# Fused delta-rule attention and two expert layers on one core: the Gram products moved ahead of the state's products in each group

## What is computed

```python
k_n = k / (norm(k) + 1e-6)
state = zeros((B, H, D, D))
for t in range(S):
    kt, vt, bt = k_n[:, :, t], v[:, :, t], beta[:, :, t, None]
    y[:, :, t] = einsum('bhd,bhde->bhe', q[:, :, t], state)
    v_old = einsum('bhde,bhd->bhe', state, kt)
    state = state + bt[..., None] * einsum('bhd,bhe->bhde', kt, vt - v_old)
```

## Time and profile before

| what | value |
|---|---|
| median of three runs | 1571.28 us |
| the profiled execution, its time | 1558.92 us |
| its span, from first to last instruction | 1557.2 us |
| mean granted TensorE clock, share of 2.4 GHz | 0.943 |
| TensorE busy | 1369.3 us, 88% |
| VectorE, ScalarE, GpSimd busy | 504.3, 479.6, 380.8 us |
| keep-busy products (line 960) | 192, 326 ns each (median) |
| starts of the transposes (line 993) in two neighbouring groups at full clock | 334.38 and 357.98 us |
| attention stage | 38 to 662 us |
| gated layer | 687 to 1134 us |
| routing, then the experts | 1134 to 1189, then to 1557 us |

### The profile page before, as it was taken

The page is one execution under the profiler, slowest core; times in us unless marked ns, Lnnn a source line. Parts: engine busy times, 40 slices in busy tenths (PEclk is TensorE's granted clock), DMA queues, the critical chain, the costliest instruction groups (busy, mean ns, idle before and its releaser), DMA issues.

```text
span 1557.2 us, 27716 instructions
## 1 busy us (share of the span) xinstructions
PE 1369.3 (88%) x10241; PEld 1096.6 (70%) x10242; DVE 504.3 (32%) x1030; ACT 479.6 (31%) x1159; POOL 380.8 (24%) x360
## 2 busy tenths in 40 slices
PE   4788888888888898869999999999915999999997
PEld 4677877777777787758888888888802555555554
DVE  1666555555565556421111111111130111111111
ACT  1454546354445454432222222212110111111110
POOL 4323222233232323112231223221242111111111
PEclk9789899899998989989999999999957999999999
DMA  3221000000000000060000000000092223331110
GB/s 120 67 67 32 22 27 22 27 22 27 23 27 22 27 22 27 7 221 1 1 1 1 1 0 0 0 0 1 0 352 111 73 77 107 119 110 37 32 30 6
DMA packets 39475, 72.75 MB, mean 47 GB/s; under 512 B 3946, under 2 KB 27538, under 8 KB 39377
## 3 DMA queue, kind: packets, MB, share of 16 engines
q1 hardware_dynamic: 33872, 55.50, 10.7%
q0 software_dynamic: 5504, 15.77, 3.0%
HBM read 55.50 MB, written 17.13 MB: 47 GB/s over the span
## 4 chain that ended last, share of the span: by engine, by line
PE 76%; DVE 9%; issue 6%; ACT 3%; POOL 2%; DMA 2%; DVEq 0%; SPq 0%; ACTq 0%; POOLq 0%
PE ps L1067 19%; PE ps L1131 11%; PE ps L1142 10%; PE ps L1078 10%; DVE BA L526 3%; PE ps L980 3%; PE ps L1010 3%; PE ps L1002 2%; PE ps L936 2%; DVE MP L545 2%; PE ps L935 2%; PE ps L1151 2%; PE ps L916 2%; DVE CT L536 1%; POOL xs_dram L469 1%
## 5 line engine op out<-in xcount | busy, mean ns | idle before, releaser
L1067 PE MATMUL ps<-xh,wgh 128*128 128x512 f32 x432 | 170.7, 395 | 12.7 <-DVE wol L624 7.0
L449 POOL TENSOR_TENSOR gl<-gp,gh 128x512 fp32r<-128x512 f32 x72 | 93.0, 1291 | 349.6 <-ACT gh L833 349.6
L636 DVE TENSOR_TENSOR gp<-sg,ps 128x512 f32<-128x512 f32 x72 | 49.5, 688 | 385.0 <-PE ps L1067 384.1
L1067 PE MATMUL ps<-xl,wgh 128*128 128x512 f32 x432 | 170.3, 394 | 0.0
L1131 PE MATMUL ps<-W,xsT 128*128 x372 | 168.6, 603 | 1.9 <-ACT xsT L884 1.0
L1067 PE MATMUL ps<-xh,wgl 128*128 128x512 f32 x432 | 169.8, 393 | 0.0
L1142 PE MATMUL ps<-W,hT 128*128 x496 | 165.1, 486 | 0.9 <-ACT hT L880 0.9
L545 DVE TENSOR_TENSOR MP<-ps,mE 128x256 f16<-128x256 f32 x288 | 115.5, 421 | 136.9 <-PE ps L1002 133.4
L1142 PEld LDWEIGHTS ps<-W,hT 128*128 128x128 f32 x496 | 94.2, 190 | 73.0 <-issue 15.5
L762 ACT CAST Xs<-ps 128x256 f16<-128x256 f32 x288 | 109.6, 381 | 98.4 <-PE ps L1010 92.8
L428 POOL TENSOR_TENSOR lof<-CT,BA 128x512 f32<-128x512 f16 x48 | 62.5, 1301 | 264.0 <-DVE CT L536 264.0
(11 more groups left out here) (177 smaller groups left out, 2446.2 us busy)
## 6 DMA issues: line engine op xcount, KB each, us to landing
W<-w_dram SPq DMA_DIRECT2D x16, 1536.0 KB, 11.0
kv<-kv_dram SPq DMA_DIRECT2D x24, 384.0 KB, 3.1
xs_dram<-zrow SPq DMA_DIRECT2D x1, 6076.0 KB, 22.0
xs<-xs_dram POOLq DMA_DIRECT2D x31, 196.0 KB, 2.7
kqT<-qT_dram SPq DMA_DIRECT2D x48, 96.0 KB, 2.5
XX<-woT_dram SPq DMA_DIRECT2D x1, 2304.0 KB, 9.9
stage<-w_gate_dram SPq DMA_DIRECT2D x6, 384.0 KB, 3.7
stage<-w_val_dram SPq DMA_DIRECT2D x6, 384.0 KB, 3.2
```

The source lines that it names most:

```text
L449: pool.tensor_tensor(gl[f % 2][:, :], gp[f % 2][:, :], gh[f % 2][:, :].bitcast(F32), ALU.subtract).then_inc(gl_ok, 1)
L636: nc.vector.tensor_tensor(gp[f % 2][:, :], sg[f % 2][:, :], ps[2 + f % 2][:, :], ALU.mult).then_inc(gp_ok, 1)
L1067: mm = pe.matmul(s[:, :], w[:, m, a, cols], v[par][:, a, :], start=(a == 0 and x == 0), stop=(a == KT - 1 and x == 2))
```

## The change

In every body that has a front and a rear, TensorE issues the Gram products first, and `keys_state(0)` and `keys_state(1)` behind them. `weights_w(0)` moves behind the transposes of the first half, `weights_w(1)` behind those of the second half. On VectorE, Rp moves from ahead of the maskings to behind the first half's XTs. All eight keep-busy products of a body are gone from there; `keep_warm` is called nowhere else. The closing body keeps its order, without keep-busy products.

```diff
--- before.py
+++ after.py
@@ -518,7 +518,7 @@
                     ins = nc.vector.tensor_tensor(sv, sv, ps[7][rows, 0:NPAIR * D].rearrange("p (h d) -> p h d", d=D), ALU.add)
                 ins.then_inc(st_ok, 1)
 
-            if cg is not None:
+            if cg is not None and g is None:
                 keys_state()
             if g is not None:
                 for j in range(4):
@@ -537,6 +537,8 @@
                         wait(dve, ct_ok, 2 * g + hf + 1)
                         wait(dve, xx_ps, 16 * g)
                         nc.vector.tensor_tensor(XTs[:, hs, :], CT[:, hs, :], mL[:, :].unsqueeze(1).to_broadcast([P, 4, P]), ALU.mult).then_inc(xt1_ok, 1)
+                        if hf == 0 and cg is not None:
+                            keys_state()
             if g is not None:
                 for l in range(1, LEVELS):
                     for hf in range(2):
@@ -965,11 +967,9 @@
                     for f, *a in chain.get((l, x), ()):
                         f(*a)
 
-            if cg is not None:
+            if cg is not None and g is None:
                 keys_state(0)
-                keep_warm(2, 0)
                 keys_state(1)
-                keep_warm(2, 0)
             if g is not None:
                 wait(pe, kT_ok, 2 * g + 2)
                 wait(pe, q_in[par], 32 * (base // 2) + 32 * (k // 2 + 1))
@@ -980,11 +980,12 @@
                         mm = pe.matmul(ps[j][:, 256 * s:256 * s + 256], kbT[:, p, r, :],
                                        kqT[par][:, p, :, :].rearrange("p a t -> p (a t)"), start=True, stop=True)
                     mm.then_inc(gram_ps, 1)
-            if cg is not None:
+            if cg is not None and g is not None:
+                keys_state(0)
+                keys_state(1)
+            if g is None:
                 weights_w(0)
-                keep_warm(4, 4)
-                if g is None:
-                    weights_w(1)
+                weights_w(1)
             if g is not None:
                 wait(pe, ba_ok, 2 * g + 2)
                 for hf in range(2):
@@ -992,8 +993,8 @@
                     for h in range(4 * hf, 4 * hf + 4):
                         mm = pe.matmul(ps[2 + hf][:, (h % 4) * P:(h % 4 + 1) * P], XTs[:, h, :], mI16[:, :], start=True, stop=True)
                     mm.then_inc(xx_ps, 1)
-                    if hf == 0 and cg is not None:
-                        weights_w(1)
+                    if cg is not None:
+                        weights_w(hf)
 
                 for l in range(1, LEVELS):
                     for hf in range(2):
```

## The result

The changed kernel takes 1651.0 us, the median of four runs (1637.5 to 1658.7), beside 1571.2 for the one before: a ratio of 1.050, with a 95% interval from 1.042 to 1.057. It is slower by 80 us. The forecast was 1618 in a range from 1578 to 1656.

What follows compares the result with a forecast made beforehand. Bound: the attention stage, losing time to waits and the clock (mean 0.92). Order, heads and closing pass -2.6 us, clock 18 x 3.9 - 7 x 3.0 = +49: +46.6 on the profiled execution, 1605.5, plus 12.4 to the median: 1618; range 1578 to 1656.

Steps and rivals of the forecast that it cites:

- The sign and the cause: Whole kernel: slower, since the granted clock falls behind TensorE's longer wait ahead of the transposes; +49 of +46.6 us, 70%.
- Gram first: Group head: Gram products start 0.94 us earlier, as 0.6 of the 1.54 removed becomes a wait for the key copy.
- the signs of the forecast: What would show it: among others, Gram products right behind the second key copy, about 0.4 us after the last exit products.
- Rp on the path: VectorE, between first XTs and third masking: Rp's 0.56 us is paid on the path, with no new wait on TensorE.
- The load behind it: SyncE issues the next keys' load after Rp, landing at 335.9 before GpSimd wants it at 337.65; cost nothing.
- The first half of the residual's products: Between the two transposes instead of under VectorE's maskings: delays the first level's dependent products, cost 0.47 us per group.
- Sum at unchanged clock: Ordinary group: -0.94 + 0.56 + 0.47 = +0.09 us; 18 such groups give +1.6 us.
- The heads of the passes: Five groups at loop-pass heads, Gram passes slow: 1.60 us won instead of 0.94, net -0.57 each, -2.9 for five.
- The number of low stretches: Granted clock at 0.50 behind the wait ahead of the transposes in 18 of 23 groups, between the 7 before and all.
- The price of one: Cost of one group's low-clock stretch: 3.9 us taken, between at least 3.0 and at most 6.0.
- The dear end of my bounds: Highest price of a low stretch, 6.0 us: slow to the exit, 4.2, plus the residual's products doubled, 1.76.
- The first of the two sections of the Trainium skill that I weighed: Basis of the second rival: a wait of 2.3 us leaves the clock as before; sum -2.6 us, 1568.7; 8%.

Runs made afterwards that it cites:

- the version with four keep-busy products: The changed kernel with four keep-busy products put into TensorE's wait ahead of the transposes, behind the keys' products: 1567.2 us, ratio 0.997 to the kernel before.
- the version with thirteen: The changed kernel with thirteen keep-busy products filling TensorE's wait ahead of the transposes, behind the keys' products: 1535.4 us, ratio 0.978 to the kernel before.
- five and two around the residual's first half: The changed kernel with the residual's first-half products back ahead of the transposes, five keep-busy products ahead of them and two behind: 1524.1 us, ratio 0.971.

## Why the prediction was right, and where it was not

**The sign and the cause** were right for the change as a whole. With the clock held the changed kernel takes 1535.4 us, and its period is that of the kernel before: no part of the 80 us is left that anything but the clock would have to explain. What the forecast did not separate are the two halves of its sum. The old order with its wait filled and the four products off its path takes 1531.3, so the order alone costs 0.6 us per ordinary group; the four products, gone from the path, pay for it.

**Gram first:** 0.94 us won was forecast, with 0.08 for the hand-over; it is 0.12, so 0.90. The new wait for the key copy is there, 0.44 on average, as the signs of the forecast had it (about 0.4). Of the 0.90, 0.6 are the four keep-busy products, which the old order can drop as well.

**Rp on the path:** 0.56 forecast, 5.35 - 4.78 = 0.57 measured, and no wait on its products.

**The load behind it:** the load is issued at T + 5.61 (400.46), forecast T + 5.6. No wait of GpSimd for it shows among the waits that matter.

**The first half of the residual's products:** 0.47 forecast; 0.4 by the periods 23.6 and 23.2 with and without.

**Sum at unchanged clock:** +0.09 us per group forecast; the period is 23.57 to 23.62 beside 23.60 (-0.90 + 0.57 + 0.4 = +0.07).

**The heads of the passes:** 0.57 won each was forecast, for five heads; the long standing (2.9 to 3.4 us) shows at four. Won are 0.9 each by the intervals less the low stretch, and 3.2 against an old order in which a second standing shows. The forecast knew only one standing; why the second costs the new order nothing was not taken apart.

**The number of low stretches:** 18 forecast, 19 found. That it came so close is luck in part: 18 was a choice between two ends, and nothing in the rows gave it. The rows were also read a little too simply: of the seven stretches before, six stand behind the wait of 1.1 us that 20 groups have, and the first does not.

**The price of one** is the term that failed. I took 3.9 us, between 3.0 from a row and an end of 6.0 for a stretch up to the exit products. Measured: a stretch is 342/19 = 18.0 us long on average, at 0.33 us for each of them: 6.0 us. The rate was nearly right (0.30); the length was not. In the rows the stretch lasted 10 us, began 2 us behind the transposes and ended in the later levels, and I took that for the usual length. In the changed kernel seventeen of the nineteen begin within 0.6 us of the transposes, with the residual's short products in them, and twelve last 20.5 us, up to the group's exit products, at 6.8 us each. The dear end of my bounds, 6.0, was the mean. The 274 low us more than before (342 - 68), at 0.33, are 90 us; the span grew by 87. The same step put the stage's mean clock near 0.8, where it is 0.73. The time lies within the range, 5 us from its top, since the range went up to the dear end; the value 1618 did not.

The clock fell behind waits of 2.18, 1.75 and 1.53 us, and of 1.10 in six groups of twenty. The first of the two sections of the Trainium skill that I weighed ("TensorE: Matmul & The Clock Gate", "HAM oscillation — how this bites in real kernels") tells of longer waits than these; as the only rule it would have left the clock alone here, and these runs contradict that. The section "A second HAM failure mode: psum-queue depth-cycling" of the same page of the Trainium skill, on frequent short idle times between groups of products in another kernel, agrees with them.

## What to carry to other kernels

Products that compute nothing can be what holds the clock: before taking them out or moving work past them, look at what the granted clock does behind the wait that they stand in. They belong into a wait that is there anyway (thirteen of them saved 116 us in the new order, six more 20 us in the old one), not on the path (there, four cost 0.6 us per group and held nothing once the wait was filled). Judge an order of work with the clock held at the same level in both versions, and with everything else equal: here the changed kernel looked 80 us worse than the one before, was 36 us better with its wait filled, and is still 4 us behind the old order with the same care taken. The sum of a change can hide a term that costs behind one that gains.

## What the runs showed of the hardware that was not expected

The granted clock falls behind short idle times: 1.1 us of wait ahead of short products was enough in 6 of the 20 groups that have it (in the kernel before), 1.75 us in all 20 (without keep-busy products). The length of the wait is not all: 0.87 and 0.18 us, with short products between them, were enough in 17 of 20.

It comes back slowly where TensorE is busy with short products: 19.4 of 20.4 us busy and still 0.50 all the time, and 10.2 us at a stretch instead of mostly 20.5 once six keep-busy products stood in the levels.

Where the clock is on the edge, runs of one kernel differ: ten runs of the version with four keep-busy products span 1550 to 1586, four of the version with thirteen 1535.1 to 1535.6. Other versions without a low stretch in their profile spread by 7 and 8 us over six runs (five and two around the residual's first half: 1521.6 to 1528.1; ten in the old order's wait: 1527.4 to 1535.4), so the clock is not shown to be the only cause.

At the head of a loop pass TensorE can stand twice for nothing that the profile shows (3.11 and 1.94 us). The second shows at all four heads of the old order with ten keep-busy products, but neither in the kernel before nor in the old order without those between the keys' products. Why was not tried.
